# Working on two hidden units at a time, with the small up matmuls of both layers side by side in the array

## The reference

```python
w = softmax(weight)                                  # 8 heads x 7 taps
out[b, s, h, g] = sum_k w[h, k] * x_pad[b, s + k, h, g]      # causal, 24 features a head
x = out.reshape(8192, 192)

h = x @ w_in1                                        # 192 -> 2048
x = (h / (1 + exp(-1.702 * h))) @ w_out1             # 2048 -> 192

h = x @ w_in2
P = a[0] + a[1]*h + a[2]*h*h + a[3]*h*h*h
Q = 1 + |b[0]|*|h| + |b[1]|*h*h
return (P / (Q + 1e-6)) @ w_out2
```

## Time and profile before

| | |
|---|---|
| median of 3 runs | 1423.31 us |
| profiled execution | 1423.74 us, span 1421.6 us |
| PE busy | 1351.4 us (95%), 4896 matmuls |
| DVE busy | 1300.1 us (91%) |
| ACT busy | 1070.3 us (75%) |
| POOL busy | 403.8 us (28%) |

### The profile page before, as it was taken

How to read it: one execution, slowest core, us unless ns; L and a number is a source line. 1 busy time by engine, 2 the same in 40 slices (tenths; PEclk the granted TensorE clock), 3 DMA queues, 4 the chain that set the end, 5 groups by cost and what they waited for, 6 DMA issues and landing times. The chain is left out here.

```text
span 1421.6 us, 18695 instructions
## 1 busy us (share of the span) xinstructions
PE 1351.4 (95%) x4896; PEld 752.5 (53%) x4896; DVE 1300.1 (91%) x1989; ACT 1070.3 (75%) x2025; POOL 403.8 (28%) x278
## 2 busy tenths in 40 slices
PE   3999999999999999999999999999999999999876
PEld 2455555555555555555555555555555555555432
DVE  5379999999999999999999999999999999998996
ACT  4377877778787877868777687777878788686885
POOL 4222232222222222222222223222222222232232
PEclk9999999999999999999999999999999999999997
DMA  8000000000000000000000000000000000000000
GB/s 222 19 12 1 12 12 1 23 1 11 11 11 11 0 22 0 11 11 0 22 0 11 11 11 11 0 22 0 11 11 11 11 0 11 0 1 12 0 12 11
DMA packets 32878, 20.28 MB, mean 14 GB/s; under 512 B 10321, under 2 KB 30801, under 8 KB 32849
## 3 DMA queue, kind: packets, MB, share of 16 engines
q1 hardware_dynamic: 32372, 19.93, 5.1%
q10 hardware_dynamic: 477, 0.01, 0.0%
HBM read 13.64 MB, written 6.29 MB: 14 GB/s over the span
## 5 line engine op out<-in xcount | busy, mean ns | idle before, releaser
L669 POOL TENSOR_TENSOR work<-work 128x512 f32<-128x512 f32 x256 | 381.2, 1489 | 970.0 <-ACT work L413 970.0
L256 PE MATMUL acc<-g,down 128*128 128x512 f32 x1024 | 491.5, 599 | 5.5 <-DVE g L579 5.3
L248 PE MATMUL h<-x_a_hi,up_a_hi 128*128 128x512 f32 x512 | 266.3, 520 | 55.1 <-DVE x_b L549 18.8
L428 ACT ACTIVATE work<-h 128x512 f32<-128x512 f32 x256 | 151.5, 592 | 200.1 <-PE h L252 200.1
L579 DVE SCALAR_TENSOR_TENSOR g<-work 128x512 f32<-128x512 f32 x256 | 286.3, 1118 | 0.1
L256 PEld LDWEIGHTS acc<-g,down 128*128 128x128 f32 x1024 | 188.3, 190 | 144.6 <-issue 112.4
L262 PE MATMUL acc<-g,down 128*64 128x512 f32 x1024 | 251.9, 609 | 0.0
L571 DVE SCALAR_TENSOR_TENSOR work<-work 128x512 f32<-128x512 f32 x256 | 207.8, 812 | 11.8 <-ACT work L405 11.2
L248 PEld LDWEIGHTS h<-x_a_hi,up_a_hi 128*128 128x128 f32 x512 | 96.2, 188 | 227.1 <-issue 164.5
L249 PE MATMUL h<-x_a_lo,up_a_hi 128*128 128x512 f32 x512 | 202.3, 395 | 0.0
L251 PE MATMUL h<-x_b,up_b_hi 128*128 128x512 f32 x512 | 202.2, 395 | 0.0
(11 more groups left out here) (75 smaller groups left out, 1066.3 us busy)
## 6 DMA issues: line engine op xcount, KB each, us to landing
out<-y_out SPq DMA_DIRECT2D x16, 384.0 KB, 2.5
x_in_a<-in_x SPq DMA_DIRECT2D x16, 256.0 KB, 2.8
down<-in_moe_w_out SPq DMA_DIRECT2D x8, 384.0 KB, 6.3
x_in_b<-in_x SPq DMA_DIRECT2D x32, 64.0 KB, 2.5
work<-in_moe_w_in SPq DMA_DIRECT2D x8, 256.0 KB, 5.8
work<-in_moe_w_in SPq DMA_DIRECT2D x16, 128.0 KB, 6.0
wts<-in_weight ACTq DMA_DIRECT2D x2, 0.4 KB
wts<-in_weight SPq DMA_DIRECT2D x2, 1.3 KB
```

The costliest lines, as they stand in the source:

```text
L248: mm(h, l.up_a_hi[:, cols], l.x_a_hi[:], start=True, stop=False)
L256: return mm(l.acc[:, 0, :], l.down[:, f, 0:P], l.g[:, f % G_SLOTS, :], start=f == 0, stop=f == STEPS - 1)
L669: tt(m[slot], sq[slot], seed, ALU.mult).then_inc(m_ready, 1)
```

## The change

- Two consecutive units make a **duo**. A tile has 8 program steps (`DUOS`), and every operation of ACT, DVE and POOL on hidden values works on 1024 columns (two PSUM banks, or two halves of an SBUF slot) where it had 512.
- Each layer's h still has two banks, but one duo fills both. There is no second pair: layer 1's next up waits for its gelu (`g1_ready`), layer 2's for the second reading by DVE (`t3_ready`).
- `up` keeps four of the five instructions of a unit. The fifth is `up_rest`: a 64-row matmul. Layer 1's takes rows 0 to 63 of the array and layer 2's takes rows 64 to 127, and they are issued in turn. `x_b` gets an order of rows that differs between the layers for it, which adds a fourth hi copy to `split_x1` (L411).
- The part-*b* down matmuls are paired between the layers (both write one bank `acc_b`), no longer between two units of a layer.
- The three tiles of x are double, and layer 1's next input is split in step 7 (`S_X1`) instead of step 0. The split of layer 2's input reads PSUM directly, so the copies L453, L455 and L567 fall away, and its lo parts come last in DVE's step 0.
- x's transposes have a bank of their own (`turned`) and are in steps 7 and 0.
- POOL's product waits for `h2_read` of the next duo, that is until ACT has made its three readings of the next h and DVE may begin its two operations that read PSUM.

```diff
-LAG_ACT1 = 1
-LAG_DOWN1 = 2
-LAG_UP2 = 19
-LAG_P = 20
-LAG_RATIO = 21
-LAG_DOWN2 = 22
+LAG_GELU = 0
+LAG_DOWN1 = 1
+LAG_UP2 = 10
+LAG_RATIO = 11
+LAG_DOWN2 = 12
...
+            def up_rest(l, d, p, k):
+                f, rows = 2 * d + k, slice(l.lo_row, l.lo_row + DB)
+                return mm(l.h[:, k, :], up_b_lo[rows, f * P:(f + 1) * P], l.x_b[rows, p, :], start=False, stop=True)
...
+            def down_b(l, d, slot, k):
+                f = 2 * d + k
+                return mm(acc_b[l.acc_row:l.acc_row + DB, :], l.down[:, f, P:D], l.g[:, slot, k, :],
+                          start=f == 0, stop=f == STEPS - 1)
...
 # PE, a step: up(L1), up(L2), then
+                for k in range(2):
+                    if live(n):
+                        last1 = up_rest(L1, s, p, k)
+                    if live(u):
+                        last2 = up_rest(L2, d2, p2, k)
...
+                    if e1 == 0:
+                        wait(pe, x2_hi_done, 2 * i)
+                        wait(pe, x2_lo_done, 2 * i)
+                    pe.wait_ge(g1_ready, v1 + 1)
...
+                    pe.wait_ge(g2_ready, v2 + 1)
+                for k in range(2):
+                    if live(v2):
+                        down_b(L2, e2, (s - LAG_DOWN2) % 2, k)
+                    if live(v1):
+                        down_b(L1, e1, (s - LAG_DOWN1) % 2, k)
+                if live(v1):
+                    down_a(L1, e1, (s - LAG_DOWN1) % 2).then_inc(g1_used, 1)
+                if live(v2):
+                    down_a(L2, e2, (s - LAG_DOWN2) % 2).then_inc(g2_used, 1)
...
 # ACT, a step: three readings of h, gelu, then
+                if s == S_ACC2 and tile_live(i - 2):
+                    act.wait_ge(g2_used, DUOS * (i - 1))
+                    wait(act, y_transposed, 2 * (i - 2))
+                    fn(y_b[0:DB, :], acc_b[0:DB, :], ACT.Copy).then_inc(acc2_read, 1)
+                    fn(y_a[:], L2.acc_a[:], ACT.Copy).then_inc(acc2_read, 1)
...
+                if s == S_X1 and tile_live(i + 1):
+                    split_x1(i + 1, 1 - p)
...
 # POOL, a step
-                    pool.wait_ge(seed_ready, u + 1)
-                    wait(pool, s2_ready, u - 1)
-                    tt(m[slot], sq[slot], seed, ALU.mult).then_inc(m_ready, 1)
+                    pool.wait_ge(seed_ready, v + 1)
+                    if live(v + 1):
+                        pool.wait_ge(h2_read, v + 2)
+                    wait(pool, s2_ready, v)
+                    tt(m, sq[(s - LAG_RATIO) % 2], seed, ALU.mult).then_inc(m_ready, 1)
```

More of the change, by code:

```diff
@@ L254, in down_a, with up @@
-            def down_a(l, f):
-                return mm(l.acc[:, 0, :], l.down[:, f, 0:P], l.g[:, f % G_SLOTS, :],
-                          start=f == 0, stop=f == STEPS - 1)
[L259 to L266, removed]
+            def up(l, d, p):
+                for k in range(2):
+                    h, cols = l.h[:, k, :], slice((2 * d + k) * P, (2 * d + k + 1) * P)
+                    mm(h, l.up_a_hi[:, cols], l.x_a_hi[:, p, :], start=True, stop=False)
+                    mm(h, l.up_a_hi[:, cols], l.x_a_lo[:, p, :], start=False, stop=False)
+                    mm(h, l.up_a_lo[:, cols], l.x_a_hi[:, p, :], start=False, stop=False)
+                    mm(h, l.up_b_hi[:, cols], l.x_b[:, p, :], start=False, stop=False)
@@ L360, in _ @@
+            with pe.Fori(0, (LAST - FIRST) // 2) as j:
+                for o in range(2):
+                    for s in range(DUOS):
+                        step(j * 2 + (FIRST + o), s, (FIRST + o) % 2)
+            for i in range(LAST, TILES + 2):
+                for s in range(DUOS):
+                    step(i, s, i % 2)
         @block.scalar
@@ L370, in _, with evacuate_x @@
             act.dma_start(par[:, 4:6], coef_b.partition_broadcast(P)).then_inc(params_loaded, 16)
-            def evacuate_x(tile, half, bank):
+            def evacuate_x(tile, half):
                 wait(act, conv_steps, NX * tile)
@@ L571, in step @@
                     stt(zv, s1, scale_c * d1, zv, ALU.add, ALU.mult).then_inc(z2_ready, 1)
-                if live(u):
-                    dve.wait_ge(t2_ready, u + 1)
-                    stt(tu, tu, par[:, 1:2], h, ALU.add, ALU.mult).then_inc(t3_ready, 1)
+                if s == S_X1 and tile_live(i + 1):
+                    split_x1(i + 1, 1 - p)
+                for op in conv[at[s]:at[s + 1]]:
+                    op().then_inc(conv_steps, 1)
                 if live(v):
@@ L636, in _ @@
             ts(root[:, 2:3], root[:, 1:2], 1.0, None, ALU.mult).then_inc(root_ready, 1)
[L637 to L638 removed]
             for i in range(FIRST):
[L640 to L647 removed]
+                tile_steps(i, i % 2)
```

456 lines of the change are left out of this document (209 added, 247 removed).

## The result

| | before | after |
|---|---|---|
| time, median | 1423.38 us | 1594.11 us |
| ratio | | 1.1195 (95% interval 1.1171 to 1.122) |
| span of the profiled execution | 1421.6 us | 1589.9 us |
| mean granted TensorE clock | 0.992 | 0.951 |

The change makes the kernel 12.0% slower (its own runs go from 1590.35 to 1596.08 us). I had forecast 1532 us with a range up to 1580: the direction and the waits came as forecast, the size didn't. 62 us are missing in the forecast.

What follows compares the result with a forecast made beforehand. PE was taken as the bound, with DVE close behind. From 1421.6 us, +4.5 for the head, +88 for thirteen tiles (91.3 against 84.5 us each) and +16 for the tail gave 1530 of span, 1532 us; range 1470 to 1580.

Steps and rivals of the forecast that it cites:

- wait of step 0, with x's second transposes: At the tile's border PE waits for layer 1's lo parts, queued on DVE behind L577: 4.7 us.
- wait of step 1: PE waits for layer 2's lo parts, DVE's last work in step 0: 2.35 us.
- wait of step 3: PE waits for g, which DVE delivers late with conv between L577 and L586: 0.5 us.
- wait of step 4: PE waits for g because ACT's squares stand behind its reading of two sums in step 3, plus conv: 2.0 us.
- wait of step 6: PE, after a transpose of y, waits for g, delayed by conv on DVE: 0.6 us.
- tile at full clock: Eight duos of PE work plus the waits and transposes, before any clock loss: 90.1 us.
- clock, a tile: Loss from PE running at 1.2 GHz for 3.5 us after the border's standstill: 1.2 us taken, 1.7 if always.
- 1, a shorter chain: The 9.2 us chain of readings, POOL, square, L577, L586 is shorter than added up: tile 84.5 to 81.7 us; 8%.
- d: Amount by which a duo's 9.2 us chain is shorter than forecast; 1.5 us gives a tile as before.
- 2, the shared ups don't overlap: The layers' row-half up matmuls on PE take four slots, not two, 0.46 us more a duo: 1577 us; 10%.
- 3, the clock holds: PE has the same waits but stays at 2.4 GHz: 1512 us; 15%.
- 4, the border's split in time: Layer 1's split at the tile's end is ready in time, other waits stay: 1456 us; 7%.

Runs made afterwards that it cites:

- warm: Kernel after, with extra throwaway matmuls filling PE's waits ahead of a tile's first up and step 1's downs; 1548.46 us.
- convlast: Kernel after, with DVE's conv steps moved behind L591 to the end of a step, instead of between L577 and L586; 1539.3 us.
- ylate: Kernel after, with ACT's two readings of layer 2's sums (L446, L447) moved behind the squares and the seed; 1568.78 us.
- x1six: convlast, plus the split of layer 1's next input moved from step 7 to step 6, conv's table ending a step earlier; 1444.22 us.
- repaired: x1six_ylate, plus layer 2's lo parts earlier on DVE, PE's wait for them split, and layer 1's part-a downs last in step 1; 1392.6 us.
- repaired_samerows: repaired, with layer 2's 64-row matmuls on layer 1's rows 0 to 63, which changes the computation; 1436.8 us.
- x1six_ylate: x1six, plus ACT's readings of layer 2's sums moved behind the seed; 1429.34 us.

## Why the prediction was right in direction and wrong in size

| step of the prediction | forecast | measured |
|---|---|---|
| a duo on PE without waits | 9.8 us | 9.8 us |
| shared ups | 2 slots | 0.66 us with the change of mode, so 2 |
| POOL's 1024 columns | 2.45 us | 2.37 |
| wait of step 0, with x's second transposes | 4.7 us | 4.7 (4.35 + 0.38) |
| wait of step 1 | 2.35 us | 2.8 |
| wait of step 3 | 0.5 us | 0.4 |
| wait of step 4 | 2.0 us | 2.1 |
| wait of step 6 | 0.6 us | 0.4 |
| tile at full clock | 90.1 us | 90.9 (warm) |
| **clock, a tile** | **1.2 us** | **4.5 to 4.7** |
| tile | 91.3 us | 95.5 |
| first up of tile 2 | 148.7 us | 158.95 |
| tail | 195 us | 189.7 |

**The mechanism was right.** With operations twice as wide and one pair of h banks a layer, the latency of a duo exceeds PE's 9.8 us wherever another piece of work stands in the chain, and it stands there in steps 0, 1, 3, 4 and 6. convlast, ylate, x1six and repaired each take one such piece out, and each takes its wait with it. Taken together they turn 12% slower into 2.1% faster, with the row sharing, the 1024 columns and the hold untouched. So none of those three slows the kernel down by itself; wide duos together with the order of the small work in their chain do.

**The step that failed is the clock.** I wrote that "3.5 us at half clock lose 1.7; I take 1.2 a tile, since one instance doesn't say that it is every one". Two faults are in it. I discounted a term for which I had a clean row and no row against it; every border cost its 1.6 us or more. And I put a clock behind the 4.7 us wait alone, as if 3.91 us were the shortest wait that can lower it. A wait of 2.8 us in step 1 did, and for twice as long: 6.8 us. Sum of the miss in the span, 60 us: (4.7 - 1.2) x 13 = 45, (90.9 - 90.1) x 13 = 10, the head 10 more than forecast, the tail 5 less. The head is another fault in the main. Tile 0 takes 52.8 us there (25.33 to 78.16), and I had 45.9. Its up matmuls start 0.43 us apart until 34.5, much as in the kernel before, which I left out; a duo of layer 1 alone takes 6.28 us and not 6.1, since it has three changes of mode too; and x's transposes weren't in the sum. Tile 1 takes 80.8 instead of 77.9, with one stretch of 3.4 us at 1.2 GHz, which is worth 1.7 at most.

The value could have been bounded from what stood in my own text: had I taken all of PE's waits above 2 us as followed by 3.5 us at half clock, the sum would have been 3 x 1.7 = 5.1 a tile, 1583 us. The rival for the clock went only downwards (it holds, 1512); none went up. The range's upper end, 1580, was drawn for the unshared ups, and nothing stood for a larger clock.

**The rivals.** 1, a shorter chain: refuted in after, where the waits of steps 0, 1 and 4 are as long as forecast or longer, so nothing is left for d. But repaired comes within 0.9 us of its floor of 80.0 us a tile. 2, the shared ups don't overlap: refuted by the 0.66 us, and priced by repaired_samerows, 44 us. 3, the clock holds: refuted; warm, which enforces it for two of three waits, still has 43 us at half clock. Half of the 156 us at 1.2 GHz, 78, taken from the span leaves 1512, the rival's number. 4, the border's split in time: refuted, L560 is behind L577; x1six shows what it would be worth, 95 us and not the 76 that I gave it, since its clock goes with it.

**The hold.** The prediction called it a cost of order whose gain is DVE time that bounds nothing. In after and in repaired DVE's g is on the path, and it costs 209 and 106 us to leave it out, the low clock behind the longer waits included. The forecast wasn't hurt, since the hold was in the walk, but the reason given was wrong.

**Open.** What decides whether low clock follows a wait, and for how long, isn't settled. The length of the wait alone doesn't. In convlast the border's wait, 4.34 us as in after, has twice the low stretch behind it, and step 1's 2.3 us has one less than 14 us later:

```profile
886.40:893.20 6.80, 5.33 (x13) 4.17 (x14) 3.70 (x5) 0.47 (x1) 0.00 (x0) 0.50 0.03 7
...
906.90:910.30 3.40, 3.23 (x8) 0.85 (x8) 3.04 (x7) 1.84 (x3) 2.36 (x1) 0.50 0.00 0
```

So an earlier low stretch doesn't protect a later wait either. In x1six_ylate only step 1's wait is left, with the same work ahead of it in every tile. Low clock follows it in five of ten tiles (752.43) and not in the other five (837.02):

```profile
752.43 2.49 PE L277 MATMUL acc_b<-g,down 128*64 128x512 f32 x8 [2.32 <-DVE x_a_lo L593]
...
837.02 1.94 PE L277 MATMUL acc_b<-g,down 128*64 128x512 f32 x8 [2.33 <-DVE x_a_lo L593]
```

No run tried a wait of set length by itself, or the same wait at another moment.

## What to carry to other kernels

Before merging units into wider operations, add the latency of one merged unit to every small operation that sits in the same in-order queue, and compare with the PE time of a unit; then move each such operation behind the one that PE waits for before judging the merge. Price a new PE wait of 2 us or more with its clock: here a wait of 4.4 us cost 6 to 7 and one of 2.8 us nearly 6. Take it for every tile in the upper bound, since the same wait was followed by low clock in some tiles and not in others. And give the clock term a rival that goes up as well as one that goes down.

## What the runs showed of the chip that I had not expected

- TensorE was granted 1.2 GHz after standstills of 2.0 to 2.8 us in the middle of dense work, and the low stretch doesn't grow with the standstill: 6.8 us behind 2.76 and 3.4 behind 4.35 in one tile of after, but 6.8 behind 4.34 and 3.4 behind 2.31 in one of convlast.
- The row halves don't depend on the order of issue: four matmuls took 0.67 us as layer 1, 1, 2, 2 and 0.66 interleaved. The Trainium skill ("TensorEngine Tiling (Array Packing)", Key Properties) says that different tiles run independently; the trace agrees, and shows that it reaches past the next instruction. On the same rows they took 1.13.
- While a POOL product of 1024 columns reads SBUF (2.4 to 2.9 us), a DVE operation with all its tensors in SBUF that starts beside it lasts until the product's end or longer, whatever its size: 1024 columns 3.42 us instead of 1.22, 256 columns 2.60 instead of 0.48, six columns 2.35. The last is a halo step (L532) with one SBUF input, so it is neither the wide operations alone nor those with two inputs.
